# Scaling attention's outputs as they leave PSUM, and other routing steps, in an attention and mixture-of-experts kernel

## The reference

```python
# attention: q, k, v of 4 x 8 x 576 x 64, s of 4 x 8 x 576
scores = q @ k.T / 8
cum = cumsum(max(s, 0))
scores = where(causal, -1e9, scores + min(cum_k - cum_q, 0))
attn = exp(scores - max(scores))
attn = attn / (sum(attn) + 1e-9)
x = (attn @ v)                       # as 2304 tokens x 512 (8 heads of 64)
# experts: each token goes to 2 of 8
noisy = x @ w_gate + log1p(exp(x @ w_noise)) * noise
out = sum over the two largest e of softmax weight * (max(x @ w1[e], 0) @ w2[e])
# last layer
y = (sigmoid(out @ w_gate2) * (out @ w_val)) @ w_out
```

## Time and profile before

| | us |
|---|---|
| median of 3 runs | 1283.97 (1282.68 to 1285.23) |
| the profiled execution | 1284.95 |
| its span | 1283.1 |
| attention, to the last weighing's end | 0 to 236 |
| routing, to the first expert product | 236 to 281.7 |
| experts and last layer | 281.7 to 1283.1 |

### The profile page before, as it was taken

One profiled execution on the slowest core, in us unless ns is written; L12 is line 12 of the kernel. 1 busy time (PEld: TensorE's weight loads), 2 busy tenths in 40 slices (PEclk: granted clock), 3 DMA queues, 4 the chain that ended last, 5 costly groups with the idle time before them and its releaser, 6 DMA issues.

```text
span 1283.1 us, 23378 instructions
## 1 busy us (share of the span) xinstructions
PE 1240.1 (97%) x7318; PEld 1074.9 (84%) x7319; DVE 504.5 (39%) x926; ACT 516.8 (40%) x1188; POOL 365.8 (29%) x406
## 2 busy tenths in 40 slices
PE   6999999789999999999999999899999999999998
PEld 5777787577888888888888888799999989999997
DVE  6788887746050506060605080522231311313211
ACT  5788888654343333433333334312122121121211
POOL 2224442005344545354535463301010100100000
PEclk7899999879999999999999999999999999999999
DMA  5533232235151664242333411302010100100000
GB/s 103 180 70 72 67 72 57 102 125 142 37 176 53 209 217 149 74 147 89 123 108 104 135 45 41 116 1 68 8 50 26 43 33 1 50 25 1 26 1 25
DMA packets 100359, 101.71 MB, mean 79 GB/s; under 512 B 70129, under 2 KB 70129, under 8 KB 100273
## 3 DMA queue, kind: packets, MB, share of 16 engines
q1 hardware_dynamic: 85168, 64.64, 17.1%
q0 software_dynamic: 7344, 20.87, 5.9%
q10 hardware_dynamic: 7792, 15.47, 3.2%
HBM read 80.06 MB, written 22.73 MB: 80 GB/s over the span
## 4 chain that ended last, share of the span: by engine, by line
PE 86%; DVE 6%; issue 4%; ACT 3%; DMA 1%; DVEq 0%; POOL 0%; ACTq 0%; POOLq 0%
PE PB L1545 10%; PE PB L1544 10%; PE PB L1543 10%; PE PD L1543 9%; PE PD L1545 9%; PE PD L1544 9%; PE PA L1543 4%; PE PA L1545 4%; PE PA L1544 4%; PE PC L1396 3%; PE PC L1578 3%; ACT xtok L880 2%; PE PB L1440 2%; DVE probT L1036 2%; PE PB L1442 1%
## 5 line engine op out<-in xcount | busy, mean ns | idle before, releaser
L1249 DVE CAST WX<-raw 128x1024 fp32r<-128x1024 f32 x56 | 58.5, 1044 | 272.7 <-DMA raw<-in_moe_w 272.7
L1292 DVE TENSOR_TENSOR gv<-sig,PB 128x384 f32<-128x384 f32 x72 | 39.9, 555 | 299.9 <-PE PB L1545 290.7
L731 POOL TENSOR_TENSOR hsTl<-hsT,hsTh 128x512 fp32r<-128x512 f32 x84 | 124.1, 1499 | 108.6 <-ACT hsT L935 108.6
L1543 PE MATMUL PB<-WX,xsTh 128*128 x344 | 137.5, 400 | 1.5 <-POOL xsTl L722 1.5
L1543 PE MATMUL PD<-WX,hsTh 128*128 x336 | 135.2, 402 | 0.0
L1545 PE MATMUL PB<-WX,xsTl 128*128 x344 | 134.9, 392 | 0.0
L1544 PE MATMUL PB<-WX,xsTh 128*128 x344 | 134.6, 391 | 0.0
L1545 PE MATMUL PD<-WX,hsTl 128*128 x336 | 131.6, 392 | 0.0
L1544 PE MATMUL PD<-WX,hsTh 128*128 x336 | 130.9, 390 | 0.0
L973 ACT ACTIVATE sig<-PA 128x384 f32<-128x384 f32 x72 | 35.4, 492 | 188.1 <-PE PA L1545 188.1
L978 ACT ACTIVATE gvh<-gv 128x384 fp32r<-128x384 f32 x72 | 37.9, 526 | 159.9 <-DVE gv L1292 157.6
(11 more groups left out here) (245 smaller groups left out, 2681.3 us busy)
## 6 DMA issues: line engine op xcount, KB each, us to landing
raw<-in_moe_w SPq DMA_DIRECT2D x28, 1024.0 KB, 5.2
y_d<-ys ACTq DMA_DIRECT2D x43, 256.0 KB
out<-fin SPq DMA_DIRECT2D x18, 256.0 KB, 2.2
qin<-in_q SPq DMA_DIRECT2D x32, 128.0 KB, 2.4
kin<-in_k SPq DMA_DIRECT2D x32, 128.0 KB, 2.5
vin<-in_v SPq DMA_DIRECT2D x32, 128.0 KB, 2.4
raw<-in_moe_w ACTq DMA_DIRECT2D x4, 1024.0 KB, 12.4
x_d<-xtok SPq DMA_DIRECT2D x16, 256.0 KB, 2.0
```

What stands on the lines that cost most here:

```text
L731: nc.gpsimd.tensor_tensor(hsTl[:, cols], hsT[:, cols], hsTh[:, cols].bitcast(F32), ALU.subtract).then_inc(hTl_done, 1)
L1249: nc.vector.tensor_copy(high, source).then_inc(w_high, 1)
L1292: nc.vector.tensor_tensor(gv[:, :], sig[:, :], PB[:, 512 * (f % 2):512 * (f % 2) + GN], ALU.mult).then_inc(gv_done, 1)
L1543: pe.matmul(acc, hi, w_hi, start=first, stop=False)
```

## The change

Sums are inverted per pair of heads: DVE does `sums` and `reciprocals` in even steps, SP stores the pair's 1/sum to a DRAM tensor `r_d` (4-byte elements, turned) and loads it back as rows spread over 64 partitions each (`RT`). PD is no longer copied by ACT but multiplied by RT on DVE (`out_scaled`). For the last pair the way is another: POOL spreads `rinv`, PE turns it, ACT copies it. Since xT is scaled, token rows need one plain ACT copy of 512 columns, all 20 on ACT, and the gate products can be summed over heads by PE (`gate_sums` with a mask `head_sum` of 16 columns). The routing arithmetic is rewritten: block and slot by adding and subtracting a rounding constant, and one-hots with 16-bit operands in wide instructions whose innermost dimension is the tile index. `keep_busy` gets (10, 16, 5) for (10, 28, 12).

```diff
-BUSY = (10, 28, 12)
+BUSY = (10, 16, 5)
...
+            def store_r(pr):
+                sp.wait_ge(r_ready, pr + 1)
...
+                sp.dma_start(r_d[heads, :].rearrange("h (j p) -> p (h j)", p=P),
+                             rinv[:, heads, :].rearrange("p h j -> p (h j)"), allow_slow_non_contiguous=True
+                             ).then_inc(r_stored, 16)
+            def load_r(pr):
+                sp.wait_ge(out_copied, pr + 1)
...
+                sp.wait_ge(r_stored, 16 * (pr + 1))
...
+                for u in range(2):
...
+                    sp.dma_start(RT[D * u:D * u + D, :], row.to_broadcast([D, S])).then_inc(r_loaded, 16)
             with sp.Fori(1, PAIRS // 2 - 1) as g_:
                 for pp in range(2):
                     load_qk(2 * g_ + pp + 1, 1 - pp)
+                    store_r(2 * g_ + pp - 2)
                     load_v(2 * g_ + pp - 1, 1 - pp)
+                    load_r(2 * g_ + pp - 2)
...
-                    copy_out()
...
             def x_row(t):
...
-                for h in range(H):
-                    last = nc.scalar.activation(xtok[t % XB][0:rows, D * h:D * h + D],
-                                                PC[0:rows, 512 * (t % 2) + D * h:512 * (t % 2) + D * h + D], ACT.Copy,
-                                                scale=rinv[0:rows, H * b + h, j:j + 1])
+                nc.scalar.activation(xtok[t % XB][0:rows, :], PC[0:rows, 512 * (t % 2):512 * (t % 2) + 512], ACT.Copy
+                                     ).then_inc(x_copied, 1)
...
+                def out_scaled():
...
+                    dve.wait_ge(weighted, pair + 2)
...
+                        dve.wait_ge(r_loaded, 32 * (pair + 1))
...
+                    nc.vector.tensor_tensor(xT[:, pair, :] if isinstance(pair, int) else
+                                            xT[:, bass.ds(pair, 1), :].rearrange("p a n -> p (a n)"),
+                                            PD[:, 0:S], RT_last if last else RT[:, :], ALU.mult
+                                            ).then_inc(out_copied, 1)
...
                     least(0)
+                    sums()
                     least(1)
+                    reciprocals()
...
                     copy(4)
+                    out_scaled()
...
-                for t in range(TT):
-                    nc.vector.tensor_scalar(ohlo[n][:, t, :], iota16[:, :], lof[:, n, t:t + 1], idc[:, t:t + 1],
-                                            ALU.is_equal, ALU.mult).then_inc(slots_ready, 1)
+                nc.vector.tensor_tensor(ohhi[n][:, :, :], block16[:, :, :], over_b(block_of[:, n, :]), ALU.is_equal
+                                        ).then_inc(blocks_made, 1)
+                if n == 0:
+                    nc.vector.tensor_tensor(ohlo[n][:, :, :], slot16[:, :, :],
+                                            slot_of[:, n, :].unsqueeze(1).to_broadcast([P, P, TT]), ALU.is_equal
+                                            ).then_inc(slots_ready, 1)
...
+            for t in (0, TT // 2):
+                nc.vector.tensor_tensor(ohlo[1][:, :, t:t + TT // 2], slot16[:, :, t:t + TT // 2],
+                                        slot_of[:, 1, t:t + TT // 2].unsqueeze(1).to_broadcast([P, P, TT // 2]),
+                                        ALU.is_equal).then_inc(slots_ready, 1)
...
+                if isinstance(hp, int) and hp == HEADS - 1:
+                    weigh_tile(1)
+                    weigh_tile(0)
+                    turn_probs(0)
+                    turn_probs(1)
+                    turn_probs(2)
+                    weigh_tile(4)
+                    weigh_tile(3)
+                    turn_last_r()
+                    turn_probs(3)
+                    turn_probs(4)
+                    gate_turned(0)
...
+                for j in range(QT):
+                    last = pe.matmul(logits[:, QT * b + j, :], gTs[b][:, P * j:P * j + P], head_sum[:, :],
+                                     start=True, stop=True, skip_group_check=True)
...
+            attention(pe, one_step)
+            for b in range(1, B):
+                gate_turned(b)
+            for b in range(B):
+                gate_sums(b)
+            for t in range(8):
+                turn_x(t)
...
             for n, upto in enumerate((17, TT)):
-                for t in range((9, 17)[n], upto):
+                for t in range((8, 17)[n], upto):
                     turn_x(t)
                 pe.wait_ge(blocks_ready, n + 1)
                 for t in range(TT):
-                    pe.wait_ge(slots_ready, TT * n + t + 1)
-                    last = pe.matmul(PB[:, 0:BLOCKS], ohlo[n][:, t, :], ohhi[n][:, t, :],
+                    pe.wait_ge(slots_ready, 1 if n == 0 else 2 + t // (TT // 2))
+                    last = pe.matmul(PB[:, 0:BLOCKS], ohlo[n][:, :, t], ohhi[n][:, :, t],
                                      start=(n + t == 0), stop=(n == 1 and t == TT - 1))
```

More of the change, by code:

```diff
@@ L468, in gate_bank @@
         def gate_bank(b):
[L469 to L475, removed]
+            return (PA, PC, PA, PD)[b]
+        logits = PB[:, 512:512 + TT * 2 * E].rearrange("p (t e) -> p t e", e=2 * E)
         def turned_in(g, u):
@@ L525, in _ @@
             load_v(0, 0)
[L527 to L530, removed]
+            for n, w in enumerate((w_gate, w_noise)):
+                sp.dma_start(Wg[:, :, E * n:E * n + E], w.rearrange("(c p) e -> p c e", p=P)).then_inc(side_loaded, 16)
             nb = noise.rearrange("(b s) e -> b s e", b=B)
@@ L1058, in least, with both, sums, reciprocals @@
                                                    op1=ALU.min, accum_out=nmax[0:rows, n:n + 1]).then_inc(masked, 1)
+                if u % 2 == 0:
+                    pr = 2 * g_ + (u - 4) // 2
+                    if isinstance(pr, int) and not 0 <= pr < PAIRS:
+                        pr = None
+                def both(x):
+                    return x[:, 2 * pr:2 * pr + 2, :] if isinstance(pr, int) else x[:, bass.ds(2 * pr, 2), :]
+                def sums():
+                    if pr is None:
+                        return
+                    dve.wait_ge(exped, QT * (2 * pr + 2))
+                    dve.sem_inc(dve_passed, 1)
+                    nc.vector.tensor_scalar(both(rinv), both(rs), 1e-9, None, ALU.add).then_inc(r_added, 1)
+                def reciprocals():
+                    if pr is None:
+                        return
+                    dve.wait_ge(r_added, pr + 1)
+                    dve.sem_inc(dve_passed, 1)
+                    nc.vector.reciprocal(both(rinv), both(rinv)).then_inc(r_ready, 1)
+                def out_scaled():
+                    if pair is None:
+                        return
+                    last = isinstance(pair, int) and pair == PAIRS - 1
+                    dve.wait_ge(weighted, pair + 2)
+                    if last:
+                        dve.wait_ge(last_r_copied, 1)
+                    else:
+                        dve.wait_ge(r_loaded, 32 * (pair + 1))
+                    dve.sem_inc(dve_passed, 1)
+                    nc.vector.tensor_tensor(xT[:, pair, :] if isinstance(pair, int) else
+                                            xT[:, bass.ds(pair, 1), :].rearrange("p a n -> p (a n)"),
+                                            PD[:, 0:S], RT_last if last else RT[:, :], ALU.mult
+                                            ).then_inc(out_copied, 1)
                 def early_high():
```

324 lines of the change are left out of this document (148 added, 176 removed).

## The result

| | before | after |
|---|---|---|
| median of the runs | 1283.33 us (1281.46 to 1285.23, 4 runs) | 1331.41 us (1326.35 to 1334.92, 4 runs) |
| span of the profiled execution | 1283.1 us | 1331.4 us |
| mean granted clock of the span | 0.979 | 0.969 |

The ratio is 1.037, with an interval of 1.035 to 1.0389: the changed kernel is 48 us slower, where 1281.5 us with a range of 1273 to 1290 was forecast.

What follows compares the result with a forecast made beforehand. TensorE was busy 97%, with attention paced by DVE's and ACT's sequence and ACT's copies holding the end. Profiled 1284.95 + 11.4 for attention - 13.9 for the tail gave 1282.4, against the median 1281.5 us; range 1273 to 1290.

Steps and rivals of the forecast that it cites:

- step (4): Attention: the sums' way through DRAM, store 8 us and loads some 3, hidden with about 5 us to spare, cost 0.
- the rival: Slow store in attention: beyond 122 ns per 4-byte piece DMA sets the pair; at 150 ns +33 us, 1314; chance 0.05.
- steps (1) to (3): Attention, DVE: `out_scaled` 0.67, `sums` and `reciprocals` 0.08, new waits and register work 0.05; together 0.80 us a pair, 14 times.
- elastic rival: Attention: the 14 multiplications cost 0.25 us each because ACT, without its copy, catches up; 1273.8 us; chance 0.15.
- (a): Behind attention, PE to the last weighing's end: gate products and turns lost, spread sums added; 10.4 us becomes 8.8.
- (b): Behind attention: three gate products, then 20 sums over heads at 0.14 us; `Abs` starts at 240.5 instead of 243.09.
- (c): Routing from Abs to scan: selection 0.36 us earlier, `ohs` 0.33 us for 0.86; scan starts at 247.4, was 252.13.
- (d): Routing from scan to first one-hot: 3.95 us instead of 4.79, so 251.35, was 256.92.
- (e): Wide one-hots on DVE: 0.5 ns a column and 0.15 fixed; first half ready at 254.0, second at 256.8.
- (f): x rows and index products on PE and ACT: last ACT copy ends at 258.25, gather at 262.0 instead of 275.03, gain 13.0.
- (g): Filling products before the first expert block: with 10 records the block starts 0.9 us sooner after the gather.
- clock rival: PE's clock falls to 1.2 GHz at the x rows (1285.8) or is still low at the first block (1291.4); chance 0.20.

Runs made afterwards that it cites:

- e3_before_store: Kernel before plus a store of each pair's sums as 1280 touching 4-byte pieces, which nobody reads or waits for: 1336.9 us, ratio 1.0384.
- e1_wide_pieces: Kernel after with the 1/sum store written as 128 pieces of 40 bytes a pair instead of 1280 of 4: 1286.39 us, ratio to before 1.0011.
- e8_gap8: Kernel before plus a store nobody waits for, 1280 4-byte pieces a pair, 8 bytes apart in the change's order: 1285.31 us, ratio 1.0001.
- e2: Kernel after without the way through DRAM (no store, loads or wait), RT set once to a constant: 1287.8 us, ratio to before 1.0022.
- e7: Kernel after without the DRAM trip, ACT again copying outputs of pairs 0 to 13, which stay unscaled: 1276.64 us, ratio to before 0.9950.
- e9_busy: Kernel after with ACT's copy, 20-byte pieces, POOL scaling, and the kernel before's filling products (28 and 12): 1280.14 us, ratio to before 0.9960.
- v2_pool_scales: Kernel after with ACT copying PD, reciprocals stored as 256 pieces of 20 bytes, POOL scaling pairs 0 to 13: 1276.79 us, ratio to before 0.9948.
- e4_spread: Kernel after with the 1280 4-byte pieces 64 bytes apart, RT loaded from a constant row: 1288.74 us, ratio to before 1.0026.

## Why the prediction was wrong, point by point

**The travel of the sums, step (4): this is the step that failed.** It put the store at 8 us, hidden, cost 0, and the rival at a chance of 0.05. The landing was not far off, 11.3 us for 8. What failed is the thought that a store of 5 KB disturbs only who waits for it. In e3_before_store nobody waits, and 52 us are lost. The spare 5 us did not hold either, since DVE waited for RT three times, 8.0 us in all. The row I scaled from, 512 pieces of 16 bytes, holds no piece below 8 bytes and so could not show the effect; the forecast had said that no trace showed a 4-byte store, and should have made that gap its largest risk. The rival's mechanism was wrong too: it asked for 122 ns a piece over all 16 DMA engines and a pair set by the sum of DMA work. DMA's share is 0.34 to 0.52 in the stretches of attention above, far from 1, and a piece took 7 ns.

The Trainium skill (DMA: Bandwidth & Descriptors, Rules for kernel authors) says that a last dimension that is not contiguous becomes one descriptor per element, and to arrange it contiguously. Doing so (e1_wide_pieces) does remove the loss. But the price is not in the number of descriptors: e8_gap8 has the same 1280 and costs nothing that can be measured (1.0001).

**DVE's added work, steps (1) to (3).** Forecast 0.80 us a pair, found 0.97: without travel a pair is 13.87 us (63.47 to 216.06 in e2, eleven pairs), for 12.90. e7 splits it: there a pair is 13.14 us, so the product is 0.73 where 0.67 was forecast, and the sums and reciprocals are 0.24 where 0.13 was. Attention is not elastic here: the product between DVE's `copy(4)` and `least(0)`, 0.67 us net of its overlap, moves the pair by 0.73. (The elastic rival's own sum was off: 0.25 us for each of 14 multiplications instead of 0.67 takes away 5.9 us, not 7.7, which gives 1275.6 for 1273.8.) These rows of e2_no_trip show the place, with no idle time between them; the second is the added one.

```profile
216.85 0.49 DVE L1056 COPY probT<-PC 128x320 f32<-128x320 f32 x1
217.26 0.75 DVE L1110 TENSOR_TENSOR xT<-PD,RT 128x576 f32<-128x576 f32 x1
217.92 0.28 DVE L1077 CUSTOM_DVE_ANT_0 scores<-PB,mask 128x128 f32<-128x128 f32 x1
```

**Behind attention.** The forecast had 42.2 us from the last exponential to the first expert product, it took 44.0 (forecast gain 13.9, found 12.0). The times to compare are those after the last exponential's end, at 225.6 before and 283.9 after, so 58.3 us are to be subtracted. PE of the kernel after, behind attention:

```profile
295.34 4.64 PE L1540 MATMUL PB<-head_sum,gTs 128*128 128x16 f32 x40
...
313.64 1.86 PE L1576 MATMUL PB<-ohhi,ohlo 128*128 128x43 f16 x20 [0.59 <-DVE ohhi L1237]
```

ACT:

```profile
300.01 0.30 ACT L920 ACTIVATE spl<-PB 128x160 f32<-128x160 f32 x1 [3.83 <-PE PB L1540]
...
311.11 1.23 ACT L906 ACTIVATE xtok<-PC 128x512 f32<-128x512 f32 x2 [0.31 <-DMA x_d<-xtok]
...
317.30 0.60 ACT L906 ACTIVATE xtok<-PC 64x512 f32<-64x512 f32 x1 [0.23 <-PE PC L1552]
```

DVE:

```profile
305.90 0.32 DVE L1198 TENSOR_TENSOR ohs<-ohk 128x160 bf16<-128x160 f32 x1
...
307.05 0.49 DVE L1204 TENSOR_TENSOR_SCAN incl<-carry,PD 128x160 f32<-128x160 f32 x1 [0.73 <-PE PD L1569]
...
311.06 0.61 DVE L1230 TENSOR_TENSOR ohhi<-block,block_of 128x860 f16<-128x860 f16 x1
311.58 1.49 DVE L1233 TENSOR_TENSOR ohlo<-slot,slot_of 128x2560 f16<-128x2560 f16 x1
```

And POOL, the first gather:

```profile
322.15 1.08 POOL L753 DMA_INDIRECT xs<-x_d,idx  x1 [23.68 <-issue]
```

- (a), (b) `Abs` at 241.7 (300.01 - 58.3), forecast 240.5. The sums over heads are the mis-sized term: 4.64 us for 20 products, 0.23 each, where 0.14 was taken from turns. That is 1.8 us more, and the rest of (a) was 0.6 better.
- (c) `ohs` takes 0.32, forecast 0.33. The scan starts at 248.75 for 247.4, the same 1.3 us late.
- (d) From scan to first one-hot 4.01 us, forecast 3.95.
- (e) 2560 columns in 1.49 us, forecast 1.45: 0.52 ns a column after the fixed 0.15, the price of the cast that the forecast took. The Trainium skill (VectorE: DVE Perf Modes, What auto-detection actually checks) gives TENSOR_TENSOR two elements a cycle if every tensor is 16-bit with step 1; the trace agrees.
- (f) The index products take 1.86 us for 20; the forecast had 0.95 and 0.3 for the spaced weights, so 0.6 too little, twice. ACT waited up to 0.3 us for the stores of x rows, which the forecast did not have. Yet the last x copy ends at 259.6 (317.90 less 58.3), forecast 258.25: nothing was added to the 1.3 us of (b). The gather follows 4.25 us later for 3.73, at 263.85, forecast 262.0.
- (g) From the first turn of the rows to the block it is 2.3 us, for 3.1 in e9_busy with the old number of filling products: 0.8 where 0.9 was forecast.

The clock rival did not come in the routing: the last row of the stretches above has 0.96. It fell in attention instead, where PE waits.

**The balance.** DVE's work is 14 x 0.97 = 13.6 us, the routing -12: near nothing, as forecast in kind, and as e1 and e2 measure it (+0.1% and +0.2%), though e2's 1287.8 lies above the 1276 to 1283 expected for it. The profiled e2 is nearer to zero than its median, 1284.03 for 1287.8: its last exponential ends 9.9 us later than before, and its routing gains 10.7. By the ratios (1.037 less 1.0011 to 1.0026) 44 to 46 of the 48 us are the store, and the rest is what the change costs without it.

## What to carry to other kernels

A DMA that nobody waits for can still stop the engines: ask of every added store what its pieces do at their destination, not only when it lands. Don't write DRAM in 4-byte pieces that lie next to each other; arrange the layout so that each partition writes 8 bytes or more in one piece (here 20 or 40), and let the reader take the strided view. Or leave a gap: starts 16, 32 and 64 bytes apart were free here, 8 bytes only in one of three orders. Work moved off one engine should go to the one with idle time at that place: DVE had none before `least(0)`, while POOL took 1.9 us of products there at no cost.

## What the runs showed of the hardware

- 4-byte pieces that touch each other in DRAM: 15 stores of 5 KB cost 52 us (e3_before_store, 1336.9 less 1284.9), 3.5 us each; split into ten stores each, 65 us. 8 bytes apart in the same order, or as touching pieces of 8 bytes (alone on the kernel before), 40 or 20 (e1_wide_pieces and v2_pool_scales): none that can be measured. 8 bytes apart in two other orders: 0.4 and 1.1%.
- The pieces of such a store pass the DMA engines as fast as spread ones: 1.8 us after the issue at 120.44 they are through, as in e4_spread after its issue at 101.50. What differs is the time until the completion, 11 us for 2.9.
- While such a store is under way ACT or DVE stops for 2 to 5 us with no wait that the trace can name, and goes on about when it lands. That the engines' code arrives behind the store is not borne out: of the packets of the kind "instruction" that the trace records, none starts between 117 and 135 us, nor between 151 and 271, while ACT's nameless waits end at 131.46, 201.70 and 234.28. What the engines wait for, and why touching pieces are slow, stays open.
- PE, turning and weighing with waits between, is granted 0.77 to 0.89 of its clock in four of the five stretches, where it had 1.00 at 96% busy. Some of the 4.2 us a pair that the store adds is this: 36 weighing products took 3.04 us at 122.5 in the middle of attention (granted 0.50, 1.2 GHz) and 1.68 at 284.97, at its end.
- Weights that PE reads in steps of 40 bytes cost 0.09 us a product, for 0.047 as the same products had in the kernel before with the weights side by side (20 in 0.94 us at 264.25, though the granted clock there was 0.50 and is 1.00 now).
